# Half-height products side by side, weight blocks in groups of four, in the dense layer of a recurrent-attention and mixture-of-experts kernel

## What is computed

```
def _moe2_ref(x, w_in, w_out):          # x: 3072 x 320, w_in: 320 x 2048, w_out: 2048 x 320
    h = x @ w_in
    g = np.maximum(0.01 * h, h)
    return (g @ w_out).astype(np.float32)
```

## Time and profile before

| | us |
|---|---|
| three runs | 804.00, 807.64, 810.27 |
| median | 807.64 |
| the profiled execution: its own time | 808.7 |
| its span in the profile | 807.0 |
| dense layer in it, first to last matmul | about 466.9 to 795.9 |

### The profile page before, as it was taken

How to read it: one execution, slowest core, us unless ns; L and a number is a source line. 1 busy time by engine, 2 the same in 40 slices (tenths; PEclk the granted TensorE clock), 3 DMA queues, 4 the chain that set the end, 5 groups by cost and what they waited for, 6 DMA issues and landing times.

```text
span 807.0 us, 17962 instructions
## 1 busy us (share of the span) xinstructions
PE 744.9 (92%) x6435; PEld 551.7 (68%) x6436; DVE 518.1 (64%) x1346; ACT 415.4 (51%) x811; POOL 192.6 (24%) x286
## 2 busy tenths in 40 slices
PE   4899999995488999999999899999999999999994
PEld 3688888885277888888888655556566555565552
DVE  6769898897887457565687565465465455554441
ACT  4578777767753458455664233343433433434332
POOL 4477787874221101111100000020100100100101
PEclk9999999998699999999999999999999999999998
DMA  6879979660527965887220000000000000000000
GB/s 195 221 232 294 326 234 340 184 203 26 176 69 266 358 219 198 262 317 256 84 83 1 2 2 1 0 34 1 25 9 2 32 0 0 32 0 0 34 1 32
DMA packets 39517, 95.87 MB, mean 119 GB/s; under 512 B 7150, under 2 KB 19630, under 8 KB 39438
## 3 DMA queue, kind: packets, MB, share of 16 engines
q1 hardware_dynamic: 31010, 66.33, 26.3%
q10 hardware_dynamic: 5788, 19.47, 6.7%
q0 software_dynamic: 2640, 9.01, 3.4%
HBM read 70.92 MB, written 23.89 MB: 117 GB/s over the span
## 4 chain that ended last, share of the span: by engine, by line
PE 83%; DVE 7%; DMA 3%; issue 3%; ACT 2%; SPq 1%; POOL 1%; ACTq 0%; DVEq 0%; POOLq 0%
PE bank L1694 34%; PE bank L1836 19%; PE bank L1728 12%; PE bank L1557 4%; PE bank L1581 4%; PE bank L1603 1%; PE bank L1684 1%; PE bank L1567 1%; PE bank L1573 1%; DMA slot<-qkT 1%; PE bank L1547 1%; DMA d_x<-og 1%; PE bank L1549 1%; PE bank L1813 1%; ACT slot L787 1%
## 5 line engine op out<-in xcount | busy, mean ns | idle before, releaser
L1694 PE MATMUL bank<-stage,slot 128*128 128x512 f16 x768 | 181.1, 379 | 0.0
L1836 PE MATMUL bank<-slot,dec 128*128 128x320 f16 x768 | 159.1, 299 | 0.0
L1694 PEld LDWEIGHTS bank<-stage,slot 128*128 128x128 f16 x768 | 75.1, 98 | 74.3 <-DVE stage L1489 0.2
L1694 PE MATMUL bank<-qbd,slot 128*128 128x128 f16 x1984 | 117.9, 221 | 7.4 <-issue 6.9
L1694 PEld LDWEIGHTS bank<-qbd,slot 128*128 128x128 f16 x1984 | 113.7, 99 | 11.0 <-issue 10.5
L1493 DVE TENSOR_TENSOR qk<-stage,dec 128x512 f16<-128x512 f32 x96 | 66.4, 692 | 84.7 <-ACT dec L989 84.7
L1836 PE MATMUL bank<-slot,qk 128*128 128x320 f16 x384 | 114.8, 299 | 0.0
L703 POOL DMA_INDIRECT out<-stage,tok_i x24 | 23.6, 983 | 368.6 <-ACT stage L1000 364.7
L989 ACT CAST dec<-stage 128x512 f16<-128x512 f32 x96 | 59.4, 619 | 100.7 <-PE bank L1836 72.0
L1489 DVE TENSOR_TENSOR stage<-bank,stage 128x512 f32<-128x512 f32 x96 | 66.2, 690 | 67.4 <-ACT stage L983 66.9
L983 ACT ACTIVATE stage<-bank 128x512 f32<-128x512 f32 x96 | 57.3, 597 | 97.5 <-PE bank L1694 96.5
(11 more groups left out here) (268 smaller groups left out, 1192.1 us busy)
## 6 DMA issues: line engine op xcount, KB each, us to landing
slot<-d_w SPq DMA_DIRECT2D x12, 1280.0 KB, 6.4
stage<-wB SPq DMA_DIRECT2D x6, 1280.0 KB, 8.3
d_w<-slot ACTq DMA_DIRECT2D x6, 1280.0 KB, 8.3
stage<-wA SPq DMA_DIRECT2D x6, 1024.0 KB, 6.5
d_w<-slot SPq DMA_DIRECT2D x4, 1280.0 KB, 8.7
stage<-wB ACTq DMA_DIRECT2D x4, 1280.0 KB, 9.3
qk<-qkT SPq DMA_DIRECT2D x12, 360.0 KB, 5.7
slot<-qkT SPq DMA_DIRECT2D x12, 360.0 KB, 8.0
```

What stands on the lines that cost most here:

```text
L1694: ins = t_.matmul(pf, a[:, col:col + P], x(k), start=(q == 0), stop=(q == len(ops) - 1))
L1836: ins = t_.matmul(bank[4 + q][:, 0:DM], x[f % 2][:, q * P:(q + 1) * P], slotB[2 + f // NF][:, c0:c0 + DM], start=(f == 0 and z == 0), stop ...
```

## The change

Four edits, all around the dense layer.

1. **Half the rows.** In weight units 8 and 9 (the dense weights), the third chunk is now laid out in two ways: blocks of the first half of the units keep the high part in rows 0 to 63 and the low part below; blocks of the second half have the low part above and the high part in rows 64 to 127. `block_at` alternates between the two kinds. The eighth matmul of a block, `f_first_end`, takes only the 64 rows that hold the high part: rows 0 to 63 for even blocks and rows 64 to 127 for odd ones.
2. **Groups of four blocks.** TensorE issues the seven full-height matmuls of four blocks (28), then the four half-height ones, then the second products of the four blocks before (48), then one token tile's turn. The four results use banks 1, 2, 3 and 0, and `fhi` and `flo` have four buffers instead of two (`ft` and `fgl` still two).
3. **Token turns** go into bank 0, which is also the fourth block's. A turn waits for that block's maximum, and the next fourth block waits for the turn's low part. The next tile's scaling stands behind the fourth block's low part on VectorE, ahead of the turned tile's low part.
4. **Written out.** The six groups stand in the program one after another on TensorE and VectorE.

```
                 sc = wsc[:, u:u + 1, k // 3]
                 if k == 2:
                     sc = wsc[KR:P, u:u + 1, 0]
+                if k == 2 and y >= NE:
+                    w, x = by_chunk(slotA[t][:, 2 * FE:3 * FE]), by_unit(part(y % 2, k))
+                    v.scalar_tensor_tensor(w[0:KR, 1, :], x[0:KR, 1, :], wsc[0:KR, u:u + 1, 0], w[0:KR, 1, :],
+                                           ALU.mult, ALU.subtract)
+                    o_ = h_ = w[KR:P, 0, :]
+                    x = x[KR:P, 0, :]
                 v.scalar_tensor_tensor(o_, x, sc, h_, ALU.mult, ALU.subtract).then_inc(lo_done, 1)
...
+            def kept_part(n, j):
+                dve.wait_ge(f_t, n + 1)
+                if n >= 2:
+                    dve.wait_ge(f_lo, n - 1)
+                v.tensor_tensor(fgl[j % 2], bank[(j + 1) % 4][:, :], ft[j % 2], ALU.max).then_inc(f_g, 1)
+
+            def first_low(n, j):
+                dve.wait_ge(f_hi, n + 1)
+                v.tensor_tensor(flo[j], fgl[j % 2], fhi[j], ALU.subtract).then_inc(f_lo, 1)
+
+            def group(gr):
+                for q in range(GT):
+                    n, t = (gr * GT + q) * 4, (gr + 1) * GT + q
+                    kept_part(n, 0)
+                    kept_part(n + 1, 1)
+                    first_low(n, 0)
+                    kept_part(n + 2, 2)
+                    first_low(n + 1, 1)
+                    kept_part(n + 3, 3)
+                    first_low(n + 2, 2)
+                    first_low(n + 3, 3)
+                    if t + 1 < NST:
+                        y_scale(t + 1, (q + 1) % GT)
+                    if t < NST:
+                        y_low(t, (gr + 1) % 2, q, 0)
...
+            def first_high(n, j):
+                act.wait_ge(f_g, n + 1)
+                if n >= 4:
+                    act.wait_ge(f_o, GT * (n - 3))
+                a.copy(fhi[j], fgl[j % 2]).then_inc(f_hi, 1)
...
+            def block_at(f):
+                return f // 2 % (NF // 2) + f % 2 * NF // 2
+
             def f_first(gr, f, i):
-                w = gr * 2 * NF + f
-                if not (isinstance(w, int) and w < 2):
-                    pe.wait_ge(f_g, w - 1)
+                n, j = gr * 2 * NF + f, f % 4
+                if n >= 4:
+                    pe.wait_ge(f_g, n - 3)
                 if f == 0:
                     pe.wait_ge(f_yl, (gr + 1) * GT)
-                first(slotA[2 + f // NF], lambda k: yh[i][:, k, :], lambda k: yl[i][:, k, :],
-                      bank[f % 2][:, :], f % NF, 512).then_inc(f_h, 1)
+                if j == 3 and 4 <= n < NST * 4 - 4 * GT + 4:
+                    pe.wait_ge(f_yl, GT + n // 4)
+                a, at, lo = slotA[2 + f // NF], block_at(f) * P, 3 * FE
+                for q, (col, x, k) in enumerate([(at, yh, 0), (lo + at, yh, 0), (at, yl, 0), (FE + at, yh, 1),
+                                                 (lo + FE + at, yh, 1), (FE + at, yl, 1), (2 * FE + at, yh, 2)]):
+                    t_.matmul(bank[(j + 1) % 4][:, :], a[:, col:col + P], x[i][:, k, :], start=(q == 0), stop=False)
+
+            def f_first_end(f, i):
+                at, r = 2 * FE + block_at(f) * P, f % 2 * KR
+                t_.matmul(bank[(f + 1) % 4][:, :], slotA[2 + f // NF][r:r + KR, at:at + P], yl[i][r:r + KR, 2, :],
+                          start=False, stop=True).then_inc(f_h, 1)
...
-            def group(gr, i, prep):
-                for f in range(2 * NF):
-                    f_first(gr, f, i)
-                    if f < 2 and not (isinstance(gr, int) and gr == 0):
-                        f_second(gr - 1, 2 * NF - 2 + f)
-                    if f >= 2:
-                        f_second(gr, f - 2)
-                    if prep and f - TURN in PREP_AT:
-                        q = PREP_AT.index(f - TURN)
-                        y_turn((gr + 1) * GT + q, q)
+            def group(gr):
+                for k in range(GT):
+                    for f in range(4 * k, 4 * k + 4):
+                        f_first(gr, f, gr % 2)
+                    for f in range(4 * k, 4 * k + 4):
+                        f_first_end(f, gr % 2)
+                    for f in range(4 * k - 4, 4 * k):
+                        if f >= 0:
+                            f_second(gr, f)
+                        elif gr:
+                            f_second(gr - 1, 2 * NF + f)
+                    if gr < NGR - 1:
+                        pe.wait_ge(f_g, (gr * GT + k) * 4 + 4)
+                        y_turn((gr + 1) * GT + k, k, 0)
```

More of the change, by code:

```diff
@@ L278, in build @@
         fgl = [room(512) for _ in range(2)]
[L279 to L280 removed]
+        fhi = [dec[i][:, 0:256].bitcast(F16) for i in range(2)] + [x[:, 0:512] for x in hh]
+        flo = [qs[i][:, :, :].rearrange("p g t -> p (g t)")[:, 0:256].bitcast(F16) for i in range(2)] + [x[:, 0:512] for x in hl]
         ob = [room(GT * DM) for _ in range(2)]
@@ L974, in y_high, with part_of @@
                 a.copy(yh[i][:, :, q * P:(q + 1) * P],
-                       bank[b0 + q % 2][:, 0:3 * P].rearrange("p (k t) -> p k t", k=3)).then_inc(f_yh, 1)
-            def group(gr, i, prep):
-                for f in range(2 * NF):
[L979 to L989, removed]
-                    if prep and f - TURN in PREP_AT:
-                        q = PREP_AT.index(f - TURN)
-                        y_high((gr + 1) * GT + q, 1 - i, q)
+                       bank[b0 and b0 + q % 2][:, 0:3 * P].rearrange("p (k t) -> p k t", k=3)).then_inc(f_yh, 1)
+            def part_of(n, j):
+                act.wait_ge(f_h, n + 1)
+                if n >= 2:
+                    act.wait_ge(f_g, n - 1)
+                a.activation(ft[j % 2], bank[(j + 1) % 4][:, :], ACT.Copy, scale=0.01).then_inc(f_t, 1)
+            def first_high(n, j):
[5 more added lines that the diff above has]
+                for q in range(GT):
+                    n = (gr * GT + q) * 4
+                    part_of(n, 0)
+                    part_of(n + 1, 1)
+                    first_high(n, 0)
+                    part_of(n + 2, 2)
+                    first_high(n + 1, 1)
+                    part_of(n + 3, 3)
+                    first_high(n + 2, 2)
+                    first_high(n + 3, 3)
+                    if gr and q == 0:
+                        rows_out(gr - 1, (gr - 1) % 2)
+                    if gr < NGR - 1:
+                        y_high((gr + 1) * GT + q, (gr + 1) % 2, q, 0)
             def rows_out(gr, i):
@@ L1005, in _ @@
             for gr in range(NGR):
-                group(gr, gr % 2, gr < NGR - 1)
+                group(gr)
             rows_out(NGR - 1, 1)
@@ L1479, in y_low @@
                 v.tensor_tensor(yl[i][:, :, q * P:(q + 1) * P],
-                                bank[b0 + q % 2][:, 0:3 * P].rearrange("p (k t) -> p k t", k=3),
+                                bank[b0 and b0 + q % 2][:, 0:3 * P].rearrange("p (k t) -> p k t", k=3),
                                 yh[i][:, :, q * P:(q + 1) * P], ALU.subtract).then_inc(f_yl, 1)
-            def group(gr, i, prep):
-                for f in range(2 * NF):
-                    w = gr * 2 * NF + f
-                    dve.wait_ge(f_t, w + 1)
-                    if not (isinstance(w, int) and w < 2):
[L1488 to L1499, removed]
@@ L1515, in _ @@
             dve.wait_ge(m_y, NPAIR + 1)
[L1516 to L1521, removed]
+            y_scale(GT, 0)
+            for gr in range(NGR):
+                group(gr)
         @block.tensor
@@ L1828, in f_second @@
                 pe.wait_ge(f_lo, w + 1)
-                if f == 0 and isinstance(gr, int) and gr == 0:
+                if w == 0:
                     pe.wait_ge(m_y, NPAIR + 1)
                 for q in range(GT):
-                    if f == 0 and not (isinstance(gr, int) and gr == 0):
+                    if f == 0 and gr:
                         pe.wait_ge(f_ob, (gr - 1) * GT + q + 1)
                     for z, (x, hl_) in enumerate(((fhi, 0), (fhi, 1), (flo, 0))):
-                        c0 = (2 * (f % NF) + hl_) * DM
-                        ins = t_.matmul(bank[4 + q][:, 0:DM], x[f % 2][:, q * P:(q + 1) * P],
+                        c0 = (2 * block_at(f) + hl_) * DM
+                        ins = t_.matmul(bank[4 + q][:, 0:DM], x[f % 4][:, q * P:(q + 1) * P],
                                         slotB[2 + f // NF][:, c0:c0 + DM], start=(f == 0 and z == 0),
@@ L1861, in _ @@
             pe.wait_ge(lo_done, lows_until(NU - 1))
[L1862 to L1868, removed]
+            for gr in range(NGR):
+                group(gr)
+            for f in range(2 * NF - 4, 2 * NF):
                 f_second(NGR - 1, f)
```

20 lines of the change are left out of this document (8 added, 12 removed).

## The result

The changed kernel takes 829.11 us (median of four runs, 827.86 to 831.90), the kernel before 808.95 us in the same comparison. The ratio is 1.0263, with a 95% interval of 1.0234 to 1.0291: 2.6% slower. The forecast was 809.5 us, no change, in a range of 801.5 to 815.0.

The account below looks back on a forecast made before the run. The dense layer was taken as bound by TensorE alone; -10.4 + 1.5 + 4.6 + 4.7 - 0.2 + 1.7 = +1.9 us gave a forecast median of 809.5 us, range 801.5 to 815.0.

Parts of the forecast that it names:

- Halves side by side: Dense layer on TensorE: four half-height products cost two full ones in each of 24 groups, -10.4 us.
- the lag: Within a pair of half-height products the second starts 0.06 us behind the first, +1.5 us over 24 groups.
- The switch: TensorE going into and out of 64-row mode costs 0.19 us per group of four blocks, +4.6 us in all.
- A group of four blocks: Dense layer on TensorE: a group with its turn takes 13.6 us, against 13.8 before.
- The stall at the first turn: TensorE waits at the first turn for the fourth maximum, with no earlier group's second products as cover: +4.7 us.
- The clock behind it: After the first group's idle time TensorE's clock falls to 1.2 GHz, 3.4 us at half speed: +1.7 us.
- Rivals A: Row-mode switches free, 64-row weights taken while the last full product streams, no lag: 801.7 to 803.4 us; chance 0.20.
- D: First group's wait covered or short, and row-mode switches free: -10.6 us, 797.0 us; chance 0.04.
- rival B: Half-height products run one after another at 0.216 us each, saving nothing while switches still cost: +10.8, 818.4 us; chance 0.10.
- Steady state: no wait, but 1.0 us of room: Later groups: the fourth maximum and bank 0 are each ready 1.0 us before TensorE needs them, so no wait.
- Rival C: VectorE and ScalarE work over 1.0 us late through bank 0; half a us in 20 groups gives 819.5 us; chance 0.04.
- no other idle time until the end: Sign for the profile after: TensorE idles only once, about 4.7 us ahead of the first turn.

Follow-up runs that it names:

- experiment 6: Experiment 2 with all four half-height products of a group of four blocks on the same 64 rows: 818.76 us, ratio 1.0142 to the kernel before.
- experiment 7: The kernel before with each block's eighth product on rows 0 to 63 alone, nothing side by side: 829.56 us, ratio 1.0258.
- Experiment 2: The changed kernel with every token turn of the next group one group of four blocks earlier: 811.04 us, ratio 1.0032 to the kernel before.
- experiment 1: The changed kernel with the turned tile's low part ahead of the next tile's scaling on VectorE: 820.79 us, ratio 1.0171 to the kernel before.
- experiment 4: The changed kernel with the four closing products on all 128 rows: 839.69 us, ratio 1.0394 to the kernel before.

## Why the prediction was wrong

**What held.** The terms of the sum were nearly right one by one. Halves side by side: forecast -10.4 + 1.5 for the lag; experiment 6 shows 10.1 us between pairs and no pairs. The switch: forecast 0.19 us, 0.20 to 0.21 in experiment 7. A group of four blocks: forecast 13.59, measured 13.54. The lag of 0.06 us within a pair was the part that was too high: in the trace the two start 0.003 us apart (498.801 and 498.804). The four halves with the way out take 0.54 us, where 0.43 + 0.06 + 0.095 = 0.59 was forecast, which is 1.2 us in 24 groups. The stall at the first turn: forecast 4.7, measured 4.76. The clock behind it: forecast +1.7, measured +1.6. Together the measured terms are -5.5 + 4.8 + 1.6 - 0.2 = +0.7, where +1.9 was forecast. Experiment 2, in which the unforeseen wait is taken away, comes nearest to the kernel that the forecast described: its layer is 1.2 us longer than before, and it runs at 811.04 us.

The rule of the Trainium skill ("TensorEngine Tiling (Array Packing)", section "Tiling Modes") that a change of mode drains the TensorE agrees with the trace in kind; the runs put the price at 0.10 us at each end for 512-column products, not the whole overlap of 0.163. Rivals A and D, both with free switches, are refuted by experiment 7 (D also by the stall of 4.76 us), and rival B, halves one after another, by experiment 6: its sum for a group, 28 x 0.216 + 0.86 + 0.19 + 6.53 + 0.33 = 13.96 us, is what halves on the same rows take (13.97).

**What failed.** The step "Steady state: no wait, but 1.0 us of room". It computed when the turned tile's low part is done, 10.4 us after the start of the second products. The trace has 512.87 and 523.27, exactly 10.4. But it held this time against one reader only, the fourth block, which wants bank 0 at 11.4. The same `f_yl` has a second reader: the first block of a group waits for all four of its tiles (`if f == 0: pe.wait_ge(f_yl, (gr + 1) * GT)`), and the last of them is turned immediately ahead of it. That reader comes at 6.53 + 0.33 = 6.86. 10.4 - 6.86 is 3.5 us, the measured wait, and without the scaling in front 1.7, the measured fifth one:

```profile
755.57 1.67 PE L1853 MATMUL bank<-stage,slot 128*128 128x512 f16 x7 [1.72 <-DVE stage L1496]
```

That waiting line stood in the diff as an unchanged one. Its cover was what the change removed: before, the turns stood behind blocks 3, 6, 9 and 12 of 16 (the fourth at `f` = 12 by `PREP_AT` and `TURN`), so three blocks of 3.36 us lay between the last turn and the group start. The new code moved them behind blocks 3, 7, 11 and 15. The forecast checked the new wait and not the old one whose distance had shrunk. Rival C priced a mistake of this kind, a round trip on VectorE that comes too late, but through bank 0 in 20 groups and at a chance of 0.04; no fourth block and no later turn waited. Of the signs that were to show the forecast wrong none names this wait; only the line "no other idle time until the end" fails.

**The sum then.** +1.9 forecast, +16.7 for five group starts, +2.6 for one clock fall make +21.2. The measured difference is 20.2 (829.11 less 808.95) and that of the layers 20.4; the sum is higher because the forecast's terms gave +1.9 where +0.7 was measured. That 807.64 + 21.2 = 828.8 lies so near the measured 829.11 is in part luck, for the kernel before took 1.3 us more in the comparison than in the three runs that the forecast stood on.

**Edit 4 and the weights.** Writing out the groups shows no wait of TensorE for instructions within the layer. On VectorE two of the 64 x 1024 low parts of 1310 ns each became a pair of 64 x 512 ones of 752 and 732 ns, and no engine waits for them. No run takes edit 4 alone back.

## What to carry to other kernels

When a step is moved later, list every wait that names its semaphore, the unchanged ones too, and compare the time it is done with the time at which each reader comes; a single edge checked is not the edge that binds. In an in-order queue, put the short instruction that another engine waits for ahead of the long one that has a whole round of slack. In this kernel half-height products pay only in pairs on different rows: a pair saves 0.216 us and the way in and out costs 0.2, so two pairs to one change of row mode save 0.21 to 0.23 us, and one pair would about break even (not run).

## What the runs showed of the hardware

**Row mode.** A 64-row product of 512 columns, alone, takes the time of a 128-row one; two in different rows and different banks run side by side: four of them, each some 0.38 us long in the profile, span 0.60 us in all. In the changed kernel they start at 498.801 and 498.804, 499.027 and 499.030, and the next full-height product at 499.338. Going in and out costs 0.2 us together, where the whole modelled overlap at both seams would be 0.33.

**The clock behind short waits.** Behind the stall of 4.3 to 5.1 us at the first turn the clock fell to 1.2 GHz in all six profiles that have it, for 1.4 to 3.0 us lost. Behind waits of 3.5 us it fell once in four in the profile of the changed kernel and four times in four in that with full-height products, for 2.6 to 2.7 us lost each time. Behind 1.7 us it fell in none of seven (five in experiment 1, one each in the changed kernel and experiment 4). With idle matmuls in the waits it did not fall at all in the layer. What decides between falling and not behind 3.5 us was not tried; a single profile shows one draw of it.
